# Attention in steps of two token tiles and four heads, with folds per step and a new order of the first stage

## The reference, cut to what matters

```python
# B, H, S, D = 4, 8, 768, 64; 24 chunks of 32 tokens; 8 memory keys per head
for c in range(S // 32):              # chunk sees 16 tokens left, 8 right, and the memory
    scores = q_c @ concat(mem_k, k[l:r]).T / 8
    a = exp(scores - max(scores)); a /= sum(a) + 1e-9
    out[c] = a @ concat(mem_v, v[l:r])
x = out.transpose(0, 2, 1, 3).reshape(4, 768, 512)
u = x + real(fft(fft(x, axis=1), axis=2))
u = u + relu(layer_norm(u) @ w_ch1) @ w_ch2          # 512 -> 2048 -> 512
h = relu(u @ w_in)                                   # 512 -> 1024
return (h * sigmoid(conv3(h)) @ w_out)               # three taps along the tokens
```

## Time and profile before

| what | value |
|---|---|
| median of 3 runs | 1052.11 us (1051.39 to 1055.18) |
| the profiled execution: its time, its span | 1052.56 us, 1050.7 us |
| instructions | 18311 |
| busy TensorE, VectorE, ScalarE, GpSimd | 982.6, 454.4, 294.3, 132.9 us |
| mean granted TensorE clock | 0.974 |
| DMA | 92.91 MB, mean 88 GB/s |

### The profile page before, as it was taken

How to read it: one execution, slowest core, us unless ns; L and a number is a source line. 1 busy time by engine, 2 the same in 40 slices (tenths; PEclk the granted TensorE clock), 3 DMA queues, 4 the chain that set the end, 5 groups by cost and what they waited for, 6 DMA issues and landing times.

```text
span 1050.7 us, 18311 instructions
## 1 busy us (share of the span) xinstructions
PE 982.6 (94%) x7896; PEld 884.8 (84%) x7896; DVE 454.4 (43%) x684; ACT 294.3 (28%) x523; POOL 132.9 (13%) x81
## 2 busy tenths in 40 slices
PE   5397986889999999999999999999999999999998
PEld 4385875879999999999999999999998797897996
DVE  3556577536332222232222323223469177194490
ACT  2235453543211111111111111113334244143241
POOL 0605416000000000000000000000014024042041
PEclk9698988989999999999999999999999999999999
DMA  8959665443020200200102002033120110301001
GB/s 316 366 185 349 226 202 185 174 150 123 9 90 1 69 22 1 91 1 31 60 0 90 0 0 90 1 91 120 41 91 1 57 64 5 115 0 40 21 1 61
DMA packets 40579, 92.91 MB, mean 88 GB/s; under 512 B 6080, under 2 KB 6208, under 8 KB 40256
## 3 DMA queue, kind: packets, MB, share of 16 engines
q1 hardware_dynamic: 36480, 82.07, 22.4%
q10 hardware_dynamic: 3456, 6.29, 1.6%
q0 software_dynamic: 576, 3.55, 0.9%
HBM read 66.74 MB, written 25.17 MB: 87 GB/s over the span
## 4 chain that ended last, share of the span: by engine, by line
PE 66%; issue 20%; POOL 6%; DVE 3%; DMA 3%; ACT 2%; ACTq 0%; SPq 0%; POOLq 0%
PE ps L785 26%; PE ps L800 25%; PE ps L524 7%; POOL g_lo L1217 6%; PE ps L1161 2%; DMA mix_scratch<-mix_sb 2%; PE ps L487 1%; PE ps L498 1%; PE ps L514 1%; PE ps L774 1%; DVE z_raw L221 1%; DMA k_win<-in_k 1%; DMA y_scratch<-u_sb 0%; DVE dve_sum L217 0%; ACT mix_sb L356 0%
## 5 line engine op out<-in xcount | busy, mean ns | idle before, releaser
L785 PE MATMUL ps<-un_hi,w 128*128 128x384 f32 x1024 | 286.8, 341 | 3.2 <-ACT mix_sb L364 3.2
L800 PE MATMUL ps<-w,h_hi 128*128 128x512 f32 x768 | 241.2, 395 | 0.0
L785 PEld LDWEIGHTS ps<-un_hi,w 128*128 128x128 f32 x1024 | 188.4, 189 | 7.7 <-ACT mix_sb L364 3.4
L761 DVE SCALAR_TENSOR_TENSOR h_lo<-ps,h_hi 128x384 fp32r<-128x384 f32 x128 | 71.2, 556 | 280.1 <-ACT h_hi L700 280.1
L785 PE MATMUL ps<-un_lo,w 128*128 128x384 f32 x512 | 172.7, 337 | 0.0
L700 ACT ACTIVATE h_hi<-ps 128x384 fp32r<-128x384 f32 x128 | 63.0, 492 | 377.4 <-PE ps L785 377.4
L800 PEld LDWEIGHTS ps<-w,h_hi 128*128 128x128 f32 x768 | 144.1, 188 | 27.5
L800 PE MATMUL ps<-w,h_lo 128*128 128x512 f32 x384 | 149.4, 389 | 0.0
L1151 PE MATMUL ps<-y_hi,v 128*128 128x384 f32 x512 | 130.7, 334 | 0.8 <-issue 0.8
L1161 PE MATMUL ps<-v,g_hi 128*128 128x512 f32 x384 | 118.8, 391 | 0.0
L1116 DVE SCALAR_TENSOR_TENSOR conv<-h_pad,taps,conv 128x768 f32<-128x768 f32 x64 | 100.5, 1570 | 2.3
(11 more groups left out here) (89 smaller groups left out, 1021.9 us busy)
## 6 DMA issues: line engine op xcount, KB each, us to landing
v_win<-in_v SPq DMA_DIRECT2D x24, 520.0 KB, 5.5
k_win<-in_k SPq DMA_DIRECT2D x24, 512.0 KB, 6.7
w_raw<-in_moe_w SPq DMA_DIRECT2D x16, 512.0 KB, 3.3
q_sb<-in_q SPq DMA_DIRECT2D x24, 256.0 KB, 5.0
x_scratch<-x_sb SPq DMA_DIRECT2D x8, 768.0 KB, 5.7
mix_scratch<-mix_sb ACTq DMA_DIRECT2D x24, 256.0 KB, 2.9
u_sb<-x_scratch SPq DMA_DIRECT2D x8, 768.0 KB, 4.6
mix_in<-mix_scratch SPq DMA_DIRECT2D x8, 768.0 KB, 6.2
```

The lines of the kernel that those rows point to most:

```text
L761: nc.vector.scalar_tensor_tensor(out=h_lo[:, m % 2, :], in0=ps[:, BH + m % 2, 0:HALF], scalar=0.0, in1=h_hi[:, m % 2, :].bitcast(F32), op0 ...
L785: last = nc.tensor.matmul(ps[:, BH + m % 2, 0:HALF], w[:, cols], x[:, par, c, :], start=(k == 0), stop=(k == 3 * ND - 1))
L800: last = nc.tensor.matmul(ps[:, BACC[s], :], h[:, m % 2, cols], w, start=(m == 0 and j == 0), stop=(m == M1T - 1 and j == 2))
```

## The change

A step now takes two token tiles (i and i+3) and four of the eight heads. Steps 0 to 2 of a batch are column group 0 (i = 0, 1, 2), steps 3 to 5 group 1. So every step holds all that one fold of half the width needs (4 operations of 128x256, split and lower of 128x512): folds 0, 1, 3, 4 run on GpSimd and 2, 5 on VectorE, right after their step. The seq products are ordered so that the first four need only group 0. `mix_sb` has six buffers; `mix_in` moves into the place of attention's inputs. x is stored in three pieces of 512 KB per batch instead of two of 768 KB. The tables are loaded behind fold0.1 on GpSimd's queue. All four order strings are new. Inputs are laid out to match ahead of the launch, with unchanged sizes. Number and shapes of TensorE's instructions are the same.

In the diff the order of ScalarE is left out: there, splits stand between the steps of their batch (`exp0.2 split0.0 keep0.2`), and the end reads `qs3.1 mirror3.1 mlp10 mk3.0` instead of `mlp10 qs3.1 mirror3.1 mk3.0`.

```diff
 NB = 3
-MIX = 3
+MIX = 6
...
 ORDER = {
     "tensor": (
         "scores0.0 scores0.1 turn0.0 values0.0 turn0.1 scores0.2 values0.1 scores0.3 turn0.2 values0.2 "
-        "turn0.3 scores0.4 values0.3 turn0.4 scores0.5 values0.4 turn0.5 scores1.0 values0.5 turn1.0 "
-        "scores1.1 turn1.1 seq0.0 seq0.1 values1.0 seq0.2 seq0.3 scores1.2 dim0.0 scores1.3 seq0.4 values1.1 "
-        "turn1.2 scores1.4 seq0.5 values1.2 seq0.6 turn1.3 seq0.7 scores1.5 values1.3 turn1.4 scores2.0 "
-        "values1.4 dim0.1 turn1.5 scores2.1 values1.5 turn2.0 mix0.0 mix0.1 mix0.2 turn2.1 values2.0 mix0.3 "
-        "scores2.2 mix0.4 values2.1 mix0.5 scores2.3 turn2.2 seq1.0 values2.2 seq1.1 scores2.4 seq1.2 turn2.3 "
-        "seq1.3 scores2.5 turn2.4 values2.3 dim1.0 turn2.5 seq1.4 scores3.0 seq1.5 values2.4 seq1.6 scores3.1 "
-        "seq1.7 values2.5 turn3.0 dim1.1 scores3.2 turn3.1 values3.0 mix1.0 mix1.1 mix1.2 values3.1 mix1.3 "
-        "mix1.4 mix1.5 scores3.3 seq2.0 turn3.2 seq2.1 scores3.4 seq2.2 turn3.3 seq2.3 scores3.5 turn3.4 "
-        "values3.2 dim2.0 values3.3 seq2.4 turn3.5 seq2.5 values3.4 seq2.6 seq2.7 values3.5 dim2.1 mix2.0 "
-        "mix2.1 mix2.2 mix2.3 mix2.4 mix2.5 seq3.0 seq3.1 mlp3 seq3.2 seq3.3 mlp5 dim3.0 mlp7 seq3.4 seq3.5 "
-        "mlp9 seq3.6 seq3.7 mlp10 dim3.1 mlp11 mix3.0 mix3.1 mix3.2 mix3.3 mix3.4 mix3.5 "
+        "turn0.3 scores0.4 values0.3 scores0.5 turn0.4 values0.4 scores1.0 turn0.5 values0.5 turn1.0 seq0.0 "
+        "seq0.1 seq0.2 seq0.3 seq0.4 seq0.5 scores1.1 values1.0 dim0.0 turn1.1 scores1.2 seq0.6 values1.1 "
+        "seq0.7 turn1.2 scores1.3 dim0.1 values1.2 scores1.4 turn1.3 values1.3 scores1.5 turn1.4 mix0.0 "
+        "mix0.1 mix0.2 values1.4 mix0.3 scores2.0 mix0.4 turn1.5 mix0.5 values1.5 scores2.1 turn2.0 seq1.0 "
+        "values2.0 seq1.1 turn2.1 seq1.2 scores2.2 seq1.3 values2.1 seq1.4 turn2.2 seq1.5 scores2.3 values2.2 "
+        "dim1.0 scores2.4 turn2.3 seq1.6 values2.3 seq1.7 scores2.5 turn2.4 dim1.1 values2.4 turn2.5 "
+        "scores3.0 mix1.0 mix1.1 mix1.2 values2.5 mix1.3 scores3.1 mix1.4 turn3.0 mix1.5 values3.0 turn3.1 "
+        "scores3.2 seq2.0 values3.1 seq2.1 turn3.2 seq2.2 seq2.3 scores3.3 values3.2 seq2.4 seq2.5 turn3.3 "
+        "scores3.4 values3.3 dim2.0 scores3.5 turn3.4 seq2.6 values3.4 turn3.5 seq2.7 values3.5 dim2.1 mix2.0 "
+        "mix2.1 mix2.2 mix2.3 mix2.4 mix2.5 seq3.0 seq3.1 seq3.2 seq3.3 mlp3 seq3.4 seq3.5 mlp5 dim3.0 mlp7 "
+        "seq3.6 seq3.7 mlp9 dim3.1 mlp10 mix3.0 mix3.1 mix3.2 mix3.3 mlp11 mix3.4 mix3.5 "
     ),
...
     "vector": (
-        "shift0.0 shift0.1 norm0.0 shift0.2 norm0.1 shift0.3 norm0.2 shift0.4 norm0.3 shift0.5 norm0.4 "
-        "shift1.0 norm0.5 fold0.2 shift1.1 lower0.2 bl0.0 bl0.1 norm1.0 bl0.2 bl0.3 shift1.2 shift1.3 cm0.0 "
-        "norm1.1 shift1.4 bl0.4 norm1.2 bl0.5 bl0.6 shift1.5 norm1.3 bl0.7 shift2.0 norm1.4 cm0.1 shift2.1 "
-        "norm1.5 fold1.2 norm2.0 shift2.2 lower1.2 norm2.1 shift2.3 norm2.2 bl1.0 bl1.1 shift2.4 bl1.2 bl1.3 "
-        "shift2.5 norm2.3 cm1.0 bl1.4 shift3.0 bl1.5 norm2.4 bl1.6 shift3.1 bl1.7 norm2.5 fold2.2 cm1.1 "
-        "norm3.0 lower2.2 shift3.2 norm3.1 shift3.3 bl2.0 shift3.4 bl2.1 bl2.2 bl2.3 shift3.5 norm3.2 cm2.0 "
-        "norm3.3 bl2.4 bl2.5 norm3.4 bl2.6 bl2.7 norm3.5 fold3.2 cm2.1 mlp0 lower3.2 mlp1 mlp2 bl3.0 bl3.1 "
-        "mlp4 mlp5 bl3.2 bl3.3 mlp6 mlp7 cm3.0 mlp8 bl3.4 bl3.5 mlp9 bl3.6 bl3.7 mlp10 cm3.1 "
+        "shift0.0 shift0.1 norm0.0 shift0.2 norm0.1 shift0.3 norm0.2 fold0.2 shift0.4 norm0.3 shift0.5 "
+        "lower0.2 norm0.4 shift1.0 norm0.5 fold0.5 lower0.5 bl0.0 bl0.1 bl0.2 bl0.3 bl0.4 bl0.5 shift1.1 "
+        "norm1.0 cm0.0 shift1.2 norm1.1 bl0.6 bl0.7 shift1.3 norm1.2 shift1.4 cm0.1 norm1.3 shift1.5 fold1.2 "
+        "norm1.4 shift2.0 norm1.5 lower1.2 shift2.1 fold1.5 bl1.0 norm2.0 bl1.1 lower1.5 bl1.2 shift2.2 bl1.3 "
+        "norm2.1 bl1.4 bl1.5 shift2.3 norm2.2 fold2.2 cm1.0 shift2.4 bl1.6 norm2.3 bl1.7 shift2.5 lower2.2 "
+        "cm1.1 norm2.4 shift3.0 norm2.5 shift3.1 fold2.5 norm3.0 shift3.2 lower2.5 norm3.1 bl2.0 bl2.1 bl2.2 "
+        "bl2.3 shift3.3 norm3.2 bl2.4 fold3.2 bl2.5 norm3.3 shift3.4 lower3.2 shift3.5 cm2.0 norm3.4 bl2.6 "
+        "bl2.7 norm3.5 fold3.5 cm2.1 lower3.5 mlp0 bl3.0 mlp1 bl3.1 mlp2 bl3.2 bl3.3 mlp4 mlp5 bl3.4 bl3.5 "
+        "mlp6 mlp7 cm3.0 mlp8 bl3.6 bl3.7 mlp9 cm3.1 mlp10 "
     ),
     "gpsimd": (
-        "fold0.0 fold0.1 lower0.0 lower0.1 fold1.0 fold1.1 lower1.0 lower1.1 fold2.0 fold2.1 lower2.0 "
-        "lower2.1 fold3.0 fold3.1 lower3.0 lower3.1 "
+        "fold0.0 fold0.1 lower0.0 lower0.1 fold0.3 fold0.4 lower0.3 lower0.4 fold1.0 lower1.0 fold1.1 "
+        "lower1.1 fold1.3 fold1.4 lower1.3 lower1.4 fold2.0 lower2.0 fold2.1 lower2.1 fold2.3 lower2.3 "
+        "fold2.4 lower2.4 fold3.0 fold3.1 lower3.0 lower3.1 fold3.3 fold3.4 lower3.3 lower3.4 "
     ),
 }
...
-    x_sb = sb("x_sb", [P, TILES, DM])
+    x_sb = sb("x_sb", [P, FOLDS, 2, 2, 2, P])
...
-    PLACE = {"seq": (0, 1, 2, 3, 6, 7, 8, 9), "dim": (4, 10), "mix": (12, 13, 14, 15, 16, 17)}
+    PLACE = {"seq": (0, 1, 2, 3, 4, 5, 8, 9), "dim": (6, 10), "mix": (12, 13, 14, 15, 16, 17)}
...
+    def block_of(g):
+        return (0, 2, 1, 3)[g // 2], g % 2
...
-    def fold(eng, api, i, n, sums, added, folded):
-        xa, xb = x_sb[:, i, :], x_sb[:, i + FOLDS, :]
-        api.tensor_tensor(sums[:, 0, :], xa, xb, ALU.add).then_inc(added, 1)
-        api.tensor_tensor(sums[:, 1, :], xa, xb, ALU.subtract).then_inc(added, 1)
+    def fold(eng, api, j, n, sums, added, folded):
+        group, i = divmod(j, FOLDS)
+        x = x_sb[:, i, :, :, group]
+        api.tensor_tensor(sums[:, 0], x[:, 0], x[:, 1], ALU.add).then_inc(added, 1)
+        api.tensor_tensor(sums[:, 1], x[:, 0], x[:, 1], ALU.subtract).then_inc(added, 1)
         eng.wait_ge(added, 2 * n + 2)
-        lo, hi = sums[:, :, 0:DM // 2], sums[:, :, DM // 2:DM]
-        api.tensor_tensor(z_raw[:, i, :, 0:DM // 2], lo, hi, ALU.add)
-        api.tensor_tensor(z_raw[:, i, :, DM // 2:DM], lo, hi, ALU.subtract).then_inc(folded, 1)
+        even, odd = z_raw[:, i, :, group * P:(group + 1) * P], z_raw[:, i, :, DM // 2 + group * P:DM // 2 + (group + 1) * P]
+        api.tensor_tensor(even, sums[:, :, 0], sums[:, :, 1], ALU.add)
+        api.tensor_tensor(odd, sums[:, :, 0], sums[:, :, 1], ALU.subtract).then_inc(folded, 1)
...
+    def await_folded(eng, b, j):
+        if j in ON_POOL:
+            eng.wait_ge(pool_folded, 4 * b + ON_POOL.index(j) + 1)
+        else:
+            eng.wait_ge(dve_folded, 2 * b + ON_DVE.index(j) + 1)
...
-            def store_x(b, half):
-                sp.wait_ge(x_ready, b * TILES + 3 * (half + 1))
-                sp.dma_start(x_dram[b, half].rearrange("(t p) d -> p t d", p=P),
-                             x_sb[:, 3 * half:3 * half + 3, :]).then_inc(st_x[half], 16)
+            def store_x(b, i):
+                sp.wait_ge(x_ready, b * TILES + FOLDS + i + 1)
+                sp.dma_start(x_dram[b, :, i].rearrange("e p (a g r) -> p e a g r", a=2, g=2), x_sb[:, i]).then_inc(st_x[i], 16)
...
-                if n >= TILES and n % TILES in (1, 4):
-                    store_x(n // TILES - 1, n % TILES // 3)
+                if n >= TILES and n % TILES < FOLDS:
+                    store_x(n // TILES - 1, n % TILES)
...
+            def load_tables():
+                pool.wait_ge(scored, 5)
+                for dst, src in ((seq_hi, seq_tab[0]), (seq_lo, seq_tab[1]), (dim_hi, dim_tab[0]), (dim_lo, dim_tab[1])):
+                    pool.dma_start(dst[:], src).then_inc(ld_tab, 16)
...
+            def folds(b, j):
+                n = 4 * b + ON_POOL.index(j)
+                pool.wait_ge(x_ready, b * TILES + j + 1)
...
+                fold(pool, nc.gpsimd, j, n, pool_sum, pool_added, pool_folded)
...
+            def lower(b, j):
+                pool.wait_ge(z_hi_ready, b * TILES + j + 1)
...
+                    pool.wait_ge(seq_done, 8 * (b - 1) + 4 * (j // FOLDS + 1))
+                nc.gpsimd.tensor_tensor(of_unit(z_lo, j), of_unit(z_raw, j), of_unit(z_hi, j).bitcast(F32), ALU.subtract
                                         ).then_inc(pool_lo_ready, 1)
...
                     folds(b, t)
+                    if (b, t) == (0, 1):
+                        load_tables()
...
-            def split(b, i):
-                if i < FOLDS - 1:
-                    act.wait_ge(pool_folded, 2 * b + i + 1)
-                else:
-                    act.wait_ge(dve_folded, b + 1)
+            def split(b, j):
+                await_folded(act, b, j)
                 if b > 0:
-                    act.wait_ge(seq_done, b * 8)
-                nc.scalar.activation(z_hi[:, i], z_raw[:, i], ACT.Copy).then_inc(z_hi_ready, 1)
+                    act.wait_ge(seq_done, 8 * (b - 1) + 4 * (j // FOLDS + 1))
+                nc.scalar.activation(of_unit(z_hi, j), of_unit(z_raw, j), ACT.Copy).then_inc(z_hi_ready, 1)
...
```

(46 more changed lines are left out.)

99 lines of the change are left out of this document (44 added, 55 removed), and 22 rows, old and new, of the table ORDER.

## The result

| | before | changed |
|---|---|---|
| median of six runs each, us | 1053.85 | **1038.24** (1035.27 to 1041.95) |
| ratio, 95% interval | | **0.9859** [0.9832, 0.9886] |
| profiled execution, its span, us | 1052.56, 1050.7 | 1041.72, 1039.6 |
| TensorE busy, idle over the span, us | 982.6, 68.1 | 982.4, 57.2 |
| VectorE, ScalarE, GpSimd busy, us | 454.4, 294.3, 132.9 | 448.6, 295.7, 138.5 |

The change makes the kernel 1.4% faster, 15.6 us. The forecast was 1031 us; the result lies inside the range.

What follows compares the result with a forecast made beforehand. Only the front up to 232 us, with TensorE's gaps in five places and low clock after them, had time to give. 33.0 us less and 12 us more made minus 21.0 us: 1031 us, range 1018 to 1045.

Steps and rivals of the forecast that it cites:

- low clock: TensorE at 1.2 instead of 2.4 GHz for some microseconds after each gap; removing gaps was to save 8.4 us of it.
- Start: First gap, batch 0: seq0.0 waits only for group 0 and the tables, starting at 46.0 instead of 52.0 us; minus 6.0 us.
- 86 to 103 us: TensorE gap at the mix copies: six buffers remove waits for stores; minus 9.9 us, low clock included.
- 134 to 139 us: TensorE gap waiting for cm1.1 behind fold2.2 on VectorE; no fold right ahead any more; minus 6.3 us.
- 171 to 188 us: TensorE gap behind the last fold ahead of cm2.1: half-width fold and no store wait at mix2; minus 6.5 us.
- 220 to 232 us: TensorE gap at mix3's last copies: mlp11 moves behind mix3.3 and covers four copies; minus 4.3 us.
- The cost of 12 us: Added waits from denser attention steps and saturated DMA queues in batches 1 to 3: plus 12 us, bounds 0 and 22.
- Six of the twelve: Batch 1's dense steps after the product block: 11.0 MB need 28 to 31 us against 23.2 us of TensorE; plus 6.
- The other six: Batches 2 and 3: 10.1 MB in some 30 us, 336 GB/s, near saturation, where TensorE waits without a releaser; plus 6.
- (a): Rival: DMA engines set the front's pace, so removed gaps return as k_win or fetch waits; 1041 us, chance 0.28.
- (b): Rival: VectorE's doubled two-SBUF-input folds and lowers are held by GpSimd on TensorE's path; slower, 1063 us, chance 0.08.
- (c): Rival: gaps merely move, the step's chain from scores over shift and exponential to turn limits the front; 1052 us, chance 0.09.

Runs made afterwards that it cites:

- the repeat: The changed kernel unaltered, measured and profiled again beside the kernel before: 1037.43 us, ratio 0.9862.
- the second: The changed kernel unaltered, measured and profiled a third time: 1035.95 us, ratio 0.9837.
- light loads: Only a quarter of each k and v tile loaded from batch 0's fourth step on: changed kernel 1026.52 us (0.9748), kernel before 1046.50 us (0.9929).

## Why the prediction was right, and what in it was not

**Direction and the gains by name: right.** The five gaps were to lose 24.6 us of idle time (6.0 + 6.0 + 4.3 + 5.8 + 2.5) and the rest of the 33.0 us in low clock. The named waits lost 24.9, 22.7 and 25.6 us in three profiles. Small slips in the sum cancel: 4.5 + 1.3 + 0.5 is 6.3 and not 6.5, and 2.5 + 2 is 4.5 and not 4.3. And the five places are not all: from 0 to 28 us TensorE is busy for 14.7 us only, over half of the idle time being waits for the first loads of k (7.2 us).
- Start: forecast 46.0 us, measured 44.55, and 43.84 in the repeat. The start of seq0.0 isn't the gain, though, since scores1.1 and turn1.1 (68 matmuls) were ahead of it before and now are behind it. TensorE's idle time ahead of seq0.0 fell from 28.5 to 21.8 us, 6.7 against the 6.0 forecast. In the first profile the last table was the last thing in, landing 15.1 us after its issue (16.9 in the earlier trace rows); in the repeat TensorE did not wait for it.
- 86 to 103 us: the copies' wait for their stores is gone. ScalarE's queue needs at most 0.39 us to issue one (4.20 before). But 3.0 us of idle time are left, and the 3.36 us stall ends just inside this stretch.
- 134 to 139 us: `m_all` no longer waits; the stall of 4.61 us at 132.57 has taken its place.
- 171 to 188 us: 3.13 us instead of 8.29. The fold ahead of cm2.1, here with it on VectorE:

```profile
170.60 1.30 DVE L228 TENSOR_TENSOR dve_sum<-x_sb 128x256 f32<-128x256 f32 x1
171.82 1.48 DVE L229 TENSOR_TENSOR dve_sum<-x_sb 128x256 f32<-128x256 f32 x1
173.34 0.42 DVE L232 TENSOR_TENSOR z_raw<-dve_sum 128x256 f32<-128x256 f32 x1
173.68 0.42 DVE L233 TENSOR_TENSOR z_raw<-dve_sum 128x256 f32<-128x256 f32 x1
```

  3.5 us from first to last, between the free 1.7 and the contended 4.7 us of the estimate, since only two of the four fell beside GpSimd's work, two lowers from 170.32 to 173.02 us. The unheld ones take 0.42 us, the estimated value.
- 220 to 232 us: the open copies cost 1.57 us (1.7 forecast). TensorE's steady run begins at 217.2 us, at 210.2 in the repeat and 213.5 in the second; I had said 211. By the same mark, its last wait for a copy, it was 227.5 before, so the 21 us forecast would be 206.5.

**The step that failed is the clock.** The terms counted 8.4 us of low clock as saved along with the idle time. TensorE's busy time fell by 0.2, 5.2 and 1.5 us. The idle time, of which 24.6 less 12, so 12.6 us, were forecast to go, fell by 10.9, 12.8 and 13.2. The prediction let each gap that goes take its low clock with it, but gave the waits that it added 12 us and no low clock of their own. The changed kernel's clock is low from 87.6 to 91.0, 132.0 to 135.4 and 138.8 to 145.6 us, each fall within 1.4 us of the end of one of the new stalls (87.30, 132.57 and 140.19), and once more from 176.4 to 183.2 us, behind the `m_all` wait that stayed.

The same waits can end with and without it. The repeat has that `m_all` wait too, 3.11 us long, and no low clock behind it: its seq matmuls there take 0.34 us and not 0.53, and the 400 matmuls from number 3400 on 55.6 instead of 58.0 us. This is the largest piece of the 5.0 us of busy time by which the two executions differ, and they are most of the 6.9 us between the two spans. Batch 0 is harder to read. Changed kernel, then repeat, each with two of its turns:

```profile
20.00:34.00 14.00, 9.80 (x379) 7.79 (x380) 9.35 (x19) 4.61 (x8) 7.68 (x10) 0.50 0.76 252
...
25.17 1.11 PE L520 MATMUL ps<-ident_sb,probs 128*128 128x128 f32 x4
...
30.70 1.11 PE L520 MATMUL ps<-ident_sb,probs 128*128 128x128 f32 x4
```

```profile
20.00:34.00 14.00, 8.67 (x379) 6.90 (x380) 9.83 (x20) 4.72 (x8) 9.02 (x13) 1.00 0.85 281
...
24.70 1.12 PE L520 MATMUL ps<-ident_sb,probs 128*128 128x128 f32 x4
...
30.19 0.66 PE L520 MATMUL ps<-ident_sb,probs 128*128 128x128 f32 x4
```

The 1.00 of the repeat is no measured full clock up to 27.1 us, where its records begin: the turn at 24.70 is as slow as the changed kernel's, the one at 30.19 is fast. So in the repeat the clock was low up to 27.1 us and again from 34.0 to 47.6, in the changed kernel up to 16.0 and again from 19.4 to 50.1 us, with the second fall inside the stall of 3.35 us that ends at 21.34. The same 379 matmuls take 9.80 us all at half clock, and 8.67 with half clock for the first half. With the clock's term at the measured 0.2 to 5.2 us instead of 8.4, the forecast's 21 us become 13 to 18; 15.6 were measured. What decides whether a wait is followed by the low clock stays open.

**The cost of 12 us: right in sum, half wrong in kind.** Waits for `k_win` and "issue" together grew by 14.2, 10.1 and 12.6 us. Six of the twelve I had charged to loads that can't keep up in batch 1, with more than 300 GB/s between 57 and 85 us. Measured are 229, 254 and 258 GB/s there (241 before), and no `k_win` wait at all later than 9 us. The other six, "saturated queues are where TensorE had its waits without a releaser", were 11.0 to 13.7 us. That the sum fits is therefore luck: one half didn't come, and the other came twice as large. I had said that I change nothing for the "issue" waits of batch 0, and this held: 11.5 us before, 10.2, 11.4 and 11.0 after. The growth is in the batches behind it, 2.9 us to 17.9, 14.0 and 15.6. What failed is that I priced these waits by the data rate and didn't ask what they are: in batches 1 and 2 the denser order now meets the same limit.

**The rivals.** (a), the DMA engines set the pace, had the right sign ("issue" grows by over 10 us) and its 1041 us lie nearer to the measured 1038 than the forecast's 1031. As a mechanism it may hold for a part: light loads take 8.5 us of "issue" out of the changed kernel and 2.8 out of the old one, and the waits are for blocks of instructions that cross the same engines. But the loads of k and v keep up, and fewer instructions at a higher data rate remove the waits. (b), the shared operands, did not come: GpSimd's operations have the sizes that were estimated, and VectorE loses less to them than before.

```profile
L310 POOL TENSOR_TENSOR z_lo<-z_raw,z_hi 128x512 fp32r<-128x512 f32 x16 | 20.5, 1294 | 20.9 <-ACT z_hi L343 20.9
L233 POOL TENSOR_TENSOR z_raw<-pool_sum 128x256 f32<-128x256 f32 x16 | 12.3, 768 | 0.0
```

The 20 fold and lower operations of VectorE took 13.8 us more than they would alone before the change, the 40 of now 5.6 us. The held ones, 1.30 and 1.48 us, last about as long as GpSimd's two lowers beside them (2.70 us together). By the operand-port rule of the Trainium skill (SBUF — State Buffer, Who interferes with whom) this is expected; the trace agrees, and shorter operations on the other engine make each hold shorter. (c), the chain of a step, is refuted: waits for the exponential fell from 10.4 us to none in the first profile and 0.6 us in the repeat, and with those for the shift and for ScalarE's copy the chain's waits are 12.3 us before and 3.6 and 5.1 after.

**What stays open.** The waits end a nearly constant time after a block's transfer, but whether that block was asked for late or was held up ahead of its transfer I can't tell. In the three large stalls behind batch 0 (those of over 3 us, ending at 87.30, 132.57 and 140.19 us) the transfer itself takes 0.96, 0.96 and 1.04 us, about the median of the whole kernel; it only starts 1.05, 2.11 and 1.07 us after TensorE has stopped, while the DMA engines are busy at shares of 0.96 to 1.12. The light loads suggest that the traffic plays a part, and no more. The orders tried changed the lengths of these waits, not their sum (25.4 to 28.1 us). How much of the gain needs the folds per step, and how much a still better order of the old steps would give, is open as well.

## What to carry to other kernels

When a gap closes, ask what now arrives in the dense stretch besides data: small matmuls use up their instruction stream in a few microseconds (here a block for every 127 of them), and its blocks share the DMA engines with the loads. Price a removed gap and an added wait alike, each with the clock that may follow it. And before a step is moved ahead on one engine, follow it through the orders of all engines: where one of them keeps the old order, the wait only changes its name, or grows.

## What was not expected of the hardware

- TensorE's instructions come in blocks of 16 KB (54 transfers, 0.88 MB, each 0.96 us in the median), one for some 127 matmuls with their weight loads, and TensorE resumes 1.2 to 1.5 us after a block has landed in all ten of its large waits without a releaser, and in the seven of the repeat. The page Runtime: NRT & Kernel Launch of the Trainium skill (Instruction fetch mechanics) tells of 16 KiB blocks and says that crossing a block's boundary is mostly hidden. The trace agrees on the blocks; hidden they are behind the front, but in it "issue" sums to 28 us, 26 of them at block boundaries, and to 8.5 us with half the small matmuls.
- The front runs at 374 GB/s from 86 to 103 us, with the 16 DMA engines busy at a share of 0.98. The 358 GB/s that the prediction cited from the Trainium skill (DMA: Bandwidth & Descriptors, Where 436 GB/s comes from) were no limit for this kernel; the measurement decides.
- Two executions of one program differ by 6.9 us in span, 5.0 of it TensorE's busy time at different clocks: the same wait of 3.1 us for `m_all` was followed by 6.8 us at half clock in one and by none in the other.
- A granted clock of 1.00 in a profile's row can mean that no record exists yet: in the first 16 to 27 us of these profiles four transposes take 1.11 us, as at half clock, where the table of stretches says 1.00.
